# First pair's seven products beside the first layer's last tile, two products between pairs' down units, x factors spread out

## What is computed

```python
scores = where(0 <= i - j < 64, q @ k.T / 8, -1e9)          # within one of 4 sequences
x = softmax(scores) @ v                                     # 2304 x 512
h = x @ moe_w_in;   g = s * relu(h)**2 + b;                  x = g @ moe_w_out
h = x @ moe2_w_in;  g = max(h, 0) + alpha * min(h, 0);       out = g @ moe2_w_out   # hidden width 2048
```

## Time and profile before

| | |
|---|---|
| median of 3 runs | 920.47 us (919.92 to 921.16) |
| the profiled execution, its own time | 921.57 us |
| its span, first to last instruction | 919.8 us |
| PE busy | 859.7 us (93%), 5484 matmuls |
| DVE / ACT / POOL busy | 522.4 (57%) / 399.4 (43%) / 36.2 us (4%) |
| DMA | 111.86 MB, mean 122 GB/s |
| chain that ended last | PE 76%, DVE 14%, ACT 5%, issue 2%, DMA 2% |

### The profile page before, as it was taken

One profiled execution on the slowest core, in us unless ns is written; L12 is line 12 of the kernel. 1 busy time (PEld: TensorE's weight loads), 2 busy tenths in 40 slices (PEclk: granted clock), 3 DMA queues, 4 the chain that ended last, 5 costly groups with the idle time before them and its releaser, 6 DMA issues.

```text
span 919.8 us, 14682 instructions
## 1 busy us (share of the span) xinstructions
PE 859.7 (93%) x5484; PEld 794.4 (86%) x5484; DVE 522.4 (57%) x1248; ACT 399.4 (43%) x959; POOL 36.2 (4%) x38
## 2 busy tenths in 40 slices
PE   5999999999999999999996998998899998999897
PEld 4899999999999999999995887877788887788786
DVE  6666555555555555554554555667556666655654
ACT  6566444444444444445543333344333344433331
POOL 5100000000000000002331000000000000000000
PEclk9999999999999999999998999998999998999999
DMA  7654323342342334117313533332553232343311
GB/s 243 209 153 118 116 98 114 116 154 79 110 136 99 121 113 153 58 69 268 110 46 115 184 108 99 121 106 82 153 201 112 84 125 81 118 146 126 115 35 69
DMA packets 50311, 111.86 MB, mean 122 GB/s; under 512 B 5568, under 2 KB 5568, under 8 KB 50240
## 3 DMA queue, kind: packets, MB, share of 16 engines
q1 hardware_dynamic: 50240, 110.92, 36.6%
HBM read 86.78 MB, written 24.12 MB: 121 GB/s over the span
## 4 chain that ended last, share of the span: by engine, by line
PE 76%; DVE 14%; ACT 5%; issue 2%; DMA 2%; SPq 1%; DVEq 0%; ACTq 0%
PE hid L443 19%; PE acc L473 19%; PE hid L494 14%; PE acc L517 12%; PE bank_x L517 4%; PE bank_y L517 4%; DVE plain_mem L1050 3%; DVE plain_mem L1061 3%; DVE split_mem L1066 2%; DVE plain_mem L1059 2%; PE bank_x L538 2%; DMA plain_mem<-factors_scratch 2%; PE bank_x L529 1%; ACT plain_mem L679 1%; ACT plain_mem L776 1%
## 5 line engine op out<-in xcount | busy, mean ns | idle before, releaser
L473 PE MATMUL acc<-split_mem,w_out 128*128 128x384 f32 x1152 | 224.2, 338 | 2.7 <-DVE split_mem L890 2.7
L443 PE MATMUL hid<-split_mem 128*128 128x384 f32 (+2 forms) x1164 | 218.8, 336 | 0.0
L494 PE MATMUL hid<-split_mem 128*128 128x384 f32 x1008 | 202.6, 339 | 6.9 <-DVE plain_mem L1050 4.9
L443 PEld LDWEIGHTS hid<-split_mem 128*128 128x128 f32 x1164 | 202.4, 190 | 2.7 <-issue 2.6
L473 PEld LDWEIGHTS acc<-split_mem,w_out 128*128 128x128 f32 x1152 | 199.8, 188 | 5.0 <-DVE split_mem L890 4.0
L494 PEld LDWEIGHTS hid<-split_mem 128*128 128x128 f32 x1008 | 181.7, 190 | 21.5 <-issue 7.9
L517 PE MATMUL acc<-w_out,split_mem 128*128 128x512 f32 x576 | 154.7, 405 | 37.2 <-DVE split_mem L1066 37.2
L1050 DVE TENSOR_TENSOR plain_mem<-hid,plain_mem 128x384 f32<-128x384 f32 x168 | 91.4, 556 | 157.4 <-PE hid L494 150.0
L756 ACT ACTIVATE split_mem<-plain_mem 128x384 fp32r<-128x384 f32 x96 | 50.2, 524 | 259.7 <-DVE plain_mem L1061 255.1
L517 PEld LDWEIGHTS acc<-w_out,split_mem 128*128 128x128 f32 x576 | 107.5, 192 | 62.4 <-DVE split_mem L1066 44.9
L885 DVE SCALAR_TENSOR_TENSOR plain_mem<-plain_mem,consts 128x384 f32<-128x384 f32 x96 | 59.5, 620 | 90.5 <-ACT plain_mem L662 90.4
(11 more groups left out here) (103 smaller groups left out, 600.8 us busy)
## 6 DMA issues: line engine op xcount, KB each, us to landing
plain_mem<-factors_scratch SPq DMA_DIRECT2D x168, 256.0 KB, 3.1
factors_scratch<-plain_mem SPq DMA_DIRECT2D x56, 256.0 KB, 2.2
plain_mem<-in_qk SPq DMA_DIRECT2D x15, 640.0 KB, 4.1
plain_mem<-in_v SPq DMA_DIRECT2D x18, 512.0 KB, 4.0
x_scratch<-plain_mem SPq DMA_DIRECT2D x6, 768.0 KB, 5.7
plain_mem<-x_scratch SPq DMA_DIRECT2D x6, 768.0 KB, 7.4
plain_mem<-in_w_in_a SPq DMA_DIRECT2D x16, 256.0 KB, 2.6
plain_mem<-in_w_out_a SPq DMA_DIRECT2D x16, 256.0 KB, 3.0
```

The lines of the kernel that those rows point to most:

```text
L443: mm = pe.matmul(hid[f % 2][:, at], w_in[:, f, wi, dc, :], x[t % 2][:, xi, dc, at], start=(dc == 0 and n == 0), stop=(dc == ND - 1 and n = ...
L473: mm = pe.matmul(acc[dc][:, 0:TILE], w_out[:, wi, f, dc * 128:(dc + 1) * 128], g[:, f % 2, gi, :], start=(f == 0 and n == 0), stop=(f == N ...
L494: mm = pe.matmul(hid[(7 * k + n) % 2][:, 0:TILE], ring[k % 2][:, wi, i, cc * 128:(cc + 1) * 128], xc[i][:, xi, cc * TILE:(cc + 1) * TILE], ...
```

## The change

It moves pair 0's seven products into the first layer's last tile: product n after `up(89 + n)`, n = 0 to 6, in `bank_x` and `bank_y`, with its sums, leaks and quarters in the steps of ScalarE and VectorE. The places of `ring`, `xc`, `gq` and the scratch of pair 0 are laid out anew for that (pair 0's scratch is the memory of `outs`, so the last `copy_out` waits for its quarters). Products 0 and 1 of pair 1 stand behind `down(94)` and behind `down(95)`. From pair 1 on, TensorE runs both products 0 and 1 of pair k ahead of `gather(k - 1, 0)`, and then product n + 2 behind gather n. VectorE does low 1 ahead of leak 2 and low 2 ahead of sum 6. The x factors and their sums are spread: one sum a step or pair, factors 0 to 3 of a new tile in the last pair of the old one, 4 to 6 in the first of the new. The rows' order starts with banks `bank_x`, `bank_y`. Factor loads are issued between the pieces' loads.

```diff
-    FACTOR_AT = (4, 5, 8, 9, 10, 11, 12)
-    FREED_BY_UP = {0: 1, 1: 3, 2: 4, 3: 6, 4: 7, 5: 9, 6: 10}
+    SUMS_AT = (3, 4, 5, 6)
+    FACTOR_AT = (4, 5, 7, 8, 9, 10, 11)
+    FREED_BY_UP = (1, 3, 4, 6, 7, 9, 10)
+    QUARTER_FREED_BY_UP = (11, 12, 13, 13)
+    PAIR_AT = NF - 2 - 7
+    ROWS = (4, 5, 3, 0, 1, 2)
...
-        ring = [halves(at, 7 * 256).rearrange("p w (i n) -> p w i n", i=7) for at in (0, 14336)]
-        xc = [halves(3584 + 1536 * i, 2 * TILE) for i in range(7)]
-        gq = [[halves(at, TILE) for at in quarters] for quarters in (
-            (19456, 20224, 20992, 21760), (17920, 18688, 22528, 23296))]
+        ring = [halves(at, 7 * 256).rearrange("p w (n c) -> p w n c", n=7) for at in (0, 17408)]
+        xc = [halves(3584 + 1536 * n, 2 * TILE) for n in range(7)]
+        gq = [[halves(at + 768 * n, TILE) for n in range(4)] for at in (14336, 20992)]
...
+        scratch = [plain_mem[:, at:at + 1152].rearrange("p (b t) -> p b t", b=3) for at in (10624, 7424)]
...
+        def product_bank(k, n):
+
+            return ((hid[0], hid[1]) if k else (bank_x, bank_y))[(7 * k + n) % 2]
...
+        def hidden(k, n):
+
+            return scratch[k > 0][:, n % 2]
...
-            for n in range(LOADS, 7 + LOADS):
-                load_factor(n)
             for n in range(NP + SLOTS, NP + NF):
                 load_piece(n)
-            store(NT - 1)
+                at = n - NP - SLOTS - 2 + LOADS
+                if LOADS <= at < LOADS + 7:
+                    load_factor(at)
...
+                    if n == 7 + LOADS + 3:
+                        store(NT - 1)
...
                 if k == 0 and n < 2:
+                    pe.wait_ge(x_lo, nth(NJ - 1))
+                elif k == 1 and n < 2:
                     pe.wait_ge(hid_read, C_A)
...
+                if k == 0 and a >= ND:
+                    pe.wait_ge(summed, 7)
...
+                n = c - (C_A - NF + PAIR_AT)
+                if 0 <= n:
+                    multiply(0, n)
+            for half in range(2):
+                down(C_A - 2, half)
+            multiply(1, 0)
+            for half in range(2):
+                down(C_A - 1, half)
+            multiply(1, 1)
             for k in range(1, NK):
+                if k > 1:
+                    multiply(k, 0)
+                    multiply(k, 1)
                 for n in range(NOB):
-                    multiply(k, n)
                     gather(k - 1, n)
-                multiply(k, NOB)
+                    if n + 2 < 7:
+                        multiply(k, n + 2)
...
+                if t == NT - 1:
+                    act.wait_ge(q_ready, 4)
...
                 if k == 0:
                     act.wait_ge(up_done, C_A - NF + 1)
                 elif k == 1:
-                    act.wait_ge(up_done, C_A - NF + 15)
+                    act.wait_ge(up_done, C_A)
...
+                if k == 0:
+                    act.wait_ge(up_done, C_A - NF + QUARTER_FREED_BY_UP[n] + 1)
+                elif k == 1 and n == 0:
+                    act.wait_ge(down_done, C_A)
+                elif n == 0:
+                    pair_left(k - 2)
+                act.activation(gq[k % 2][n][:, 0, :], hidden(k, n), ACT.Copy).then_inc(q_hi, 1)
...
+                    if 1 <= i < NF - 1:
                         split(NP + i - 1)
-                    if i in (2, 3):
-                        for n in range(4 * (i - 2), min(4 * (i - 1), 7)):
-                            keep_factor(n)
+                    if 3 <= i < 10:
+                        keep_factor(i - 3)
                     if i in FACTOR_AT:
                         factor_high(0, FACTOR_AT.index(i))
-            for k in range(NK):
+                    n = i - PAIR_AT - 1
+                    if n == 0:
+                        copy_first(0)
+                    if n == 2:
+                        quarter_high(0, 0)
+                    if n == 5:
+                        quarter_high(0, 1)
+                    if n == 6:
+                        keep_factor(7)
+                        quarter_high(0, 2)
+            for n in range(8, 11):
+                keep_factor(n)
+            quarter_high(0, 3)
+            for k in range(1, NK):
                 tt, c = divmod(k, PER)
+                last, new = tt < NW - 1 and c == PER - 1, tt > 0 and c == 0
                 copy_first(k)
-                if tt < NW - 1 and c == PER - 1:
+                if k == 3:
+                    split(NP + NF - 2)
+                    split(NP + NF - 1)
+                if k == 1:
+                    copy_out(NT - 1)
+                    for n in range(4, 7):
+                        keep_factor(7 + n)
+                if last:
                     factor_high(tt + 1, 0)
-                if tt > 0 and c == 0:
-                    factor_high(tt, 3)
+                    factor_high(tt + 1, 1)
+                if new:
                     factor_high(tt, 4)
                 quarter_high(k, 0)
+                if new:
+                    rows_copied(tt - 1, 0)
+                    factor_high(tt, 5)
                 if k + 1 < NK:
                     for n in range(4):
                         keep_factor(7 * (k + 1) + n)
-                if tt < NW - 1 and c == PER - 1:
-                    factor_high(tt + 1, 1)
-                if tt > 0 and c == 0:
-                    factor_high(tt, 5)
+                if last:
+                    factor_high(tt + 1, 2)
+                if new:
+                    rows_copied(tt - 1, 1)
                     factor_high(tt, 6)
-                    rows_copied(tt - 1, 0)
-                    rows_copied(tt - 1, 1)
-                if k == 0:
-                    copy_out(NT - 1)
+                    rows_copied(tt - 1, 2)
+                if last:
+                    factor_high(tt + 1, 3)
                 quarter_high(k, 1)
                 if k + 1 < NK:
                     for n in range(4, 7):
                         keep_factor(7 * (k + 1) + n)
-                if tt < NW - 1 and c == PER - 1:
-                    factor_high(tt + 1, 2)
-                if tt > 0 and c == 0:
-                    rows_copied(tt - 1, 2)
+                if new:
                     rows_copied(tt - 1, 3)
                 quarter_high(k, 2)
-                quarter_high(k, 3)
-                if k == 0:
-                    split(NP + NF - 1)
-                if tt > 0 and c == 0:
+                if new:
                     rows_copied(tt - 1, 4)
                     rows_copied(tt - 1, 5)
+                quarter_high(k, 3)
...
+            def factor_sum(tt, n):
...
-                    if i == 3:
-                        factor_sums(0)
-                    if i == 6:
-                        last_sum(0)
+                    if i in SUMS_AT:
+                        factor_sum(0, SUMS_AT.index(i))
                     if i in FACTOR_AT:
                         factor_low(0, FACTOR_AT.index(i))
-            for k in range(NK):
+                    n = i - PAIR_AT - 1
+                    if n == 1:
+                        sum_up(0, 0)
+                        leak(0, 0)
+                    if n == 2:
+                        sum_up(0, 1)
+                        quarter_low(0, 0)
+                    if n == 3:
+                        sum_up(0, 2)
+                    if n == 4:
+                        sum_up(0, 3)
+                        leak(0, 1)
+                    if n == 5:
+                        sum_up(0, 4)
+                        sum_up(0, 5)
+                        quarter_low(0, 1)
+                        leak(0, 2)
+                    if n == 6:
+                        sum_up(0, 6)
+                        leak(0, 3)
+                        quarter_low(0, 2)
+            quarter_low(0, 3)
+            copy_out(NT - 1)
+            for k in range(1, NK):
                 tt, c = divmod(k, PER)
+                last, new = tt < NW - 1 and c == PER - 1, tt > 0 and c == 0
                 sum_up(k, 0)
                 leak(k, 0)
-                if tt > 0 and c == 0:
-                    factor_low(tt, 3)
+                if last:
+                    factor_low(tt + 1, 0)
+                    factor_low(tt + 1, 1)
+                if new:
+                    factor_low(tt, 4)
+                if tt < NW - 1 and c == 4:
+                    factor_sum(tt + 1, 0)
+                if tt < NW - 1 and c == 5:
+                    factor_sum(tt + 1, 1)
+                if tt < NW - 1 and c == 6:
+                    factor_sum(tt + 1, 2)
                 sum_up(k, 1)
                 quarter_low(k, 0)
-                if tt < NW - 1 and c == PER - 1:
-                    factor_low(tt + 1, 0)
-                if tt > 0 and c == 0:
-                    factor_low(tt, 4)
+                if last:
+                    factor_sum(tt + 1, 3)
+                    factor_low(tt + 1, 2)
+                if new:
+                    factor_low(tt, 5)
                 sum_up(k, 2)
```

(52 more changed lines are left out.)

52 lines of the change are left out of this document (16 added, 36 removed).

## The result

The changed kernel takes 858.86 us (median of 4 runs, 856.81 to 859.72) against 920.19 (4 runs): a ratio of 0.9336, 95% interval 0.9308 to 0.9365. Forecast were 859.0 and a range of 855.5 to 873. The profiled execution took 858.94 us with a span of 857.2.

The account below looks back on a forecast made before the run. TensorE was taken to bound both layers. Gains 14.8 + 47.0 + 0.3 less costs 0.3 and 0.4 give 61.4 us: span 919.8 to 858.4, 860.2 for this execution, 859.0 against the median; range 855.5 to 873.

Parts of the forecast that it names:

- (a): Last tile and pair 0: gain of 12.9 us up to the first gather plus 1.9 for the restart, 14.8 us.
- SyncE's queue: Factor loads between pieces in the last tile, store(5) in pair 1: loads have 12 us against 3.1 to landing; no cost.
- Two costs of 0.3 and 0.4: Possible wait with restart: 0.3 us at pair 1's product 0 for keep_factor(7), 0.4 at the last pair's first gather.
- the square: Last tile, steps 4 to 6: VectorE's added sum and factor push the next square back some 0.9 of 1.5 us slack.
- The rule on the shared port: VectorE instructions with two SBUF inputs contend with GpSimd: up to 7.7 us over six last-tile steps, nothing while slack lasts.
- (b): Steady pairs: period falls from 17.17 to 15.64 us, a gain of 47.0 us, new tiles' 10.9 included.
- The new limit: Next pair's product 1 overwrites the bank sum 6 reads: slack 0.57 us; as rival 15 us, 874 in all, chance 0.12.
- (c): New tiles: spreading the x factors leaves nothing of the 10.9 us lost there, a gain already counted in the steady pairs.
- (d): The end, from the last pair's first gather to the span's end: unchanged but for a 0.26 us restart, gain 0.3.
- The 1.53 of a pair: Stall in each old steady pair: a wait of 1.23 us, the rest a restart with the next step 0.3 longer.

Follow-up runs that it names:

- pair 0 late: Changed kernel with pair 0's seven products back around the last two down units, its other work behind the last unit, new banks kept: 860.82 us, ratio 0.9355.
- the store moved: Kernel before with only the new order inside pairs, plus the last tile's store issued behind factor load 14, not ahead of 11: 875.72 us, ratio 0.9520.
- two instructions more: Changed kernel with leak 2's first half done three times in pairs 1 to 23, two more dependent VectorE instructions of 0.46 us: 870.06 us, ratio 0.9460.
- VectorE's order back: Changed kernel with VectorE's old order inside the pairs (low 2 behind sum 6), TensorE's order as changed: 859.61 us, ratio 0.9333.
- the pairs' order alone: Kernel before with only the new order inside the pairs, on TensorE and VectorE; pair 0, layout and x factors as before: 880.98 us, ratio 0.9563.
- the x factors lumped: Changed kernel with x factors and sums at the two new tiles in their old places on ScalarE and VectorE: 863.46 us, ratio 0.9378.

## Why the prediction was right

**(a) Last tile and pair 0.** From `down(80)` to the first gather 71.76 us were added up (488.73 - 416.97), and it took 71.85 (416.07 to 487.92). The gain's size is right. Its cause was told as the place of the products and their work, and the runs divide it otherwise: 2.3 of 14.8 by the place (pair 0 late), 2.15 by the stalls within the last tile, which are gone in the changed kernel and in pair 0 late too, 3.9 by the store's place in SyncE's queue (the store moved, in another setting of the order). The other some 6.5, by difference, no run takes apart by cause, but the rows say where they lay. In the kernel before, from `up(95)` to product 0 of pair 1 are 493.45 - 475.28 = 18.17 us for 13.52 of steps: 4.65 of waits of pair 0's products, for the last ReLU, for `copy_first` and for sums. In pair 0 late the same steps take 486.34 - 472.81 = 13.53, with the products in the same places but in `bank_x` and `bank_y`. So these 4.65 came not with the place but with the banks or the order of ScalarE's and VectorE's work. The gap behind them, up to the second gather, cost 8.0 (504.92 - 493.45 = 11.47 for 3.47 of steps, the slow restart included); 3.9 of it are the store and 2.3 the place, and 1.8 stay open. The size could be right without the cause, since the steps after the change were added up and the old time was read. The prediction costed SyncE's queue at nothing, which is right for the queue after, but didn't name what the queue before had cost, though the chain of waits of the kernel before shows it, from the store to the load behind it, and ScalarE's timeline the `keep_factor` that waited for that load:

```profile
491.73 0.33 SPq L292
...
493.54 5.33 DMA plain_mem<-factors_scratch
```
```profile
497.59 1.93 ACT L740 ACTIVATE split_mem<-plain_mem 128x512 fp32r<-128x512 f32 x3 [4.67 <-DMA plain_mem<-factors_scratch]
```

Two costs of 0.3 and 0.4 were set for ends within 0.1 us. `keep_factor(7)` cost 0.1 (484.80 - 481.59 = 3.21 for 3.12), and the last pair's first gather nothing: it starts 1.38 after the gather ahead of it (845.55 - 844.17).

In steps 4 to 6 the square was to be late by some 0.9; it is late by 0.5 to 1.0, and TensorE doesn't wait.

**The rule on the shared port** holds in the changed kernel. VectorE's timeline of step 12, beside GpSimd's instruction of 1.29 us at 472.75, and of pair 3, where the two splits left over run on GpSimd (520.11 to 522.78):

```profile
473.30 0.95 DVE L1102 TENSOR_SCALAR plain_mem<-plain_mem,consts 128x384 f32<-128x384 f32 x1
```
```profile
520.22 1.40 DVE L1102 TENSOR_SCALAR plain_mem<-plain_mem,consts 128x384 f32<-128x384 f32 x1
521.65 1.54 DVE L1104 SCALAR_TENSOR_TENSOR plain_mem<-plain_mem 128x384 f32<-128x384 f32 x1
```

The leak's first half takes 0.42 elsewhere and its second 0.56, so two instructions lose 2.0 us in pair 3. The first half has one SBUF tensor as input, beside a factor per partition; the Trainium skill (SBUF — State Buffer, Who interferes with whom) counts `tensor_scalar` among those that can take the shared pair, and the prediction had used only its clause on two inputs. TensorE lost nothing by it, in the last tile as forecast, and none in pair 3, of which the prediction said nothing (the period stays 15.64).

**(b) Steady pairs.** The period is 15.64, as added up. The new limit was named rightly. VectorE's timeline of pair 2, whose product 5 starts at 512.25 and after which product 1 of pair 3 starts at 518.16:

```profile
513.49 1.02 DVE L1093 TENSOR_TENSOR plain_mem<-hid,plain_mem 128x384 f32<-128x384 f32 x2 [0.82 <-PE hid L508]
514.43 0.55 DVE L1109 TENSOR_TENSOR split_mem<-plain_mem,split_mem 128x384 fp32r<-128x384 f32 x1
...
516.97 0.55 DVE L1093 TENSOR_TENSOR plain_mem<-hid,plain_mem 128x384 f32<-128x384 f32 x1
```

Sum 6 ends 516.97 + 0.55 - 512.25 = 5.27 after product 5's start (5.3 worked out), which leaves 0.64 for 0.57. Not all of it can be used: with two instructions more, where product 1 does wait, it starts 0.15 after sum 6's end, and 0.64 - 0.15 is the 0.48 or so of that run. The prediction had no term for this passage, and the slack was large enough without it. What the prediction said too much of is VectorE's order: it told both halves of the change as one step, and the run with VectorE's order back shows that TensorE's order alone brings the gain. By the prediction's own chain, low 2 in the old order would be ready at about 5.9, ahead of the gather at 6.9.

**(c) New tiles.** 0 were to be left of 10.9, and 0 are left (15.64 a pair). Its stated cause, the factors in a lump, holds for the 2.6 of each 5.4 that the pairs' order alone leaves; the other 2.8 went with that order.

**(d) and the sum.** The span was to be 858.4 and is 857.2. Of the 1.2 us, 0.9 are in the start of the first layer (`down(80)` at 416.07 for 416.97), which the change doesn't touch (0.86 of it stands already at 35.08 for 35.94). The costs of 0.3 and 0.4, which came to 0.1 and 0, are 0.6 more, and against that stands (d)'s gain of 0.3, which didn't come: from the last pair's first gather to the end are 11.65 us, and were 11.64. The prediction took 0.26 of a restart off there, and for the steady pairs it read the gather's step to the next product as 0.3 longer. In its rows that step is 521.02 - 519.52 = 1.50 for 1.39, and in the last pair 1.49 both before and after. The 1.53 of a pair are right as a sum, but they are a standstill of 1.40, of which the bracket shows 1.23, and 0.13 of slower steps. That the median came within 0.2 us of the forecast is thus partly luck: starts of attention that differ by up to 3.7 us between profiled executions move it by more.

## What to carry to other kernels

Where one engine's steps have fixed costs, add them up without their waits; then follow each chain that the new order leaves in hundredths of a us, and name the wait that is next, here a bank that a later sum still reads. Count a long gap back to its first link before its cause is told: a transfer in a queue, ahead of one that is wanted sooner, was worth more than the move of seven products. An order that reaches the result sooner can leave less slack for the wait that decides: two instructions more cost 12.5 us with sum 6 behind low 2, and 2.55 with it ahead (1.05 of them the old order's own), where no pair waited. And where two runs differ by a few us, take the distance between two marks in the trace before the medians: an earlier stretch can be longer or shorter by as much.

## What the runs showed of the hardware that was not expected

A short wait costs more than its bracket. A gather with a bracket of 0.17 us costs 0.47, one with 1.23 costs 1.53, both at full clock, and a product with 0.26 costs 0.52. Of the 0.3 between, 0.17 is the drain, which the bracket leaves out, and 0.13 are slower steps behind the wait (0.09 with the product). So even waits too short to matter in the list of waits are worth removing when there are 22 of them.

The same wait can cost more still. With the x factors lumped, both new tiles have brackets of 0.31 and 1.72; behind the first one's the granted clock stayed at 1.00 and they cost 2.5 us, behind the second one's it was 0.52 for a while and they cost 4.1. With the store moved it was the first tile that fell (0.57). No run shows what decides it.
